# The opening of a fused attention and two-layer kernel: order of loads, places for weight tiles and keys, order of states, and idle products

## What is computed

```python
f = 1.0 / (1.0 + np.exp(-f_logit))
state = np.zeros((B, H, D, D))
for t in range(S):
    state = f[:, :, t, :, None] * state + np.einsum('bhd,bhe->bhde', k[:, :, t], v[:, :, t])
    y[:, :, t] = np.einsum('bhd,bhde->bhe', q[:, :, t], state)
x = y.transpose(0, 2, 1, 3).reshape(3072, 384)

h = x @ w_in;  g = max(h, 0) ** 2;              x2 = g @ w_out        # first layer
h = x2 @ w_in2; g = h * tanh(log1p(exp(h)));    out = g @ w_out2      # second layer
```

## Time and profile before

| | us |
|---|---|
| median of three runs | 935.17 |
| lowest and highest of them | 934.47, 936.77 |
| the profiled execution's own time | 935.64 |
| its span, first to last instruction | 933.9 |
| TensorE matmuls busy | 908.5 (97%) |
| TensorE weight loads busy | 773.7 (83%) |
| VectorE busy | 581.7 (62%) |
| ScalarE busy | 598.6 (64%) |
| GpSimd busy | 54.0 (6%) |

### The profile page before, as it was taken

How to read it: one execution, slowest core, us unless ns; L and a number is a source line. 1 busy time by engine, 2 the same in 40 slices (tenths; PEclk the granted TensorE clock), 3 DMA queues, 4 the chain that set the end, 5 groups by cost and what they waited for, 6 DMA issues and landing times.

```text
span 933.9 us, 15574 instructions
## 1 busy us (share of the span) xinstructions
PE 908.5 (97%) x5952; PEld 773.7 (83%) x5952; DVE 581.7 (62%) x1011; ACT 598.6 (64%) x1029; POOL 54.0 (6%) x48
## 2 busy tenths in 40 slices
PE   5799999999999999999999999999999999999998
PEld 3587888888878788887788799999999899999987
DVE  7656524523443443242133599898898898898886
ACT  5566654545545455553456787787787787877875
POOL 0111111101210111110000000000000000000000
PEclk9999999999999999999999999999999999999999
DMA  6533422112121121200223400200101001000000
GB/s 183 157 122 119 129 71 82 43 41 76 42 77 40 42 82 42 71 18 1 70 68 101 135 1 1 68 1 17 52 1 34 35 0 35 35 1 1 35 1 35
DMA packets 30353, 50.62 MB, mean 54 GB/s; under 512 B 3266, under 2 KB 14530, under 8 KB 30274
## 3 DMA queue, kind: packets, MB, share of 16 engines
q1 hardware_dynamic: 30274, 49.56, 17.0%
HBM read 40.11 MB, written 9.44 MB: 53 GB/s over the span
## 4 chain that ended last, share of the span: by engine, by line
PE 94%; DVE 2%; ACT 1%; issue 1%; DVEq 0%; ACTq 0%
PE ps L897 42%; PE ps L949 21%; PE ps L912 21%; PE ps L881 3%; PE ps L858 3%; PE ps L877 2%; PE ps L887 1%; PE ps L847 1%; DVE w_lo L673 0%; DVE work L711 0%; DVE work L718 0%; DVE g_lo L722 0%; DVE work L708 0%; DVE work L652 0%; ACT yo L480 0%
## 5 line engine op out<-in xcount | busy, mean ns | idle before, releaser
L897 PE MATMUL ps<-xs,w_hi 128*128 128x512 f32 x1152 | 363.7, 397 | 8.8 <-DVE w_lo L673 4.6
L897 PEld LDWEIGHTS ps<-xs,w_hi 128*128 128x128 f32 x1152 | 212.1, 188 | 53.0 <-issue 5.1
L690 DVE TENSOR_TENSOR g_lo<-gb,g_hi 128x512 fp32r<-128x512 f32 x96 | 70.2, 732 | 261.5 <-ACT gb L471 261.5
L897 PE MATMUL ps<-xs,w_lo 128*128 128x512 f32 x576 | 227.0, 394 | 0.0
L466 ACT ACTIVATE rb<-ps 128x512 f32<-128x512 f32 x96 | 57.4, 598 | 152.5 <-PE ps L897 152.5
L949 PE MATMUL ps<-w_hi,g_hi 128*128 128x384 f32 x384 | 129.4, 337 | 0.9 <-DVE g_lo L722 0.9
L949 PE MATMUL ps<-w_hi,g_lo 128*128 128x384 f32 x384 | 129.5, 337 | 0.0
L949 PE MATMUL ps<-w_lo,g_hi 128*128 128x384 f32 x384 | 128.9, 336 | 0.0
L897 PEld LDWEIGHTS ps<-xs,w_lo 128*128 128x128 f32 x576 | 108.5, 188 | 23.7
L912 PE MATMUL ps<-g_hi,w_hi 128*128 128x512 f32 x288 | 112.4, 390 | 0.0
L912 PE MATMUL ps<-g_lo,w_hi 128*128 128x512 f32 x288 | 112.3, 390 | 0.0
(11 more groups left out here) (59 smaller groups left out, 1091.0 us busy)
## 6 DMA issues: line engine op xcount, KB each, us to landing
work<-fkq SPq DMA_DIRECT2D x72, 224.0 KB, 3.7
work<-v_tok SPq DMA_DIRECT2D x24, 256.0 KB, 3.5
stage<-w_in SPq DMA_DIRECT2D x32, 192.0 KB, 2.4
stage<-w_out SPq DMA_DIRECT2D x32, 192.0 KB, 2.6
x_scratch<-yo SPq DMA_DIRECT2D x6, 768.0 KB, 3.5
xs<-x_scratch SPq DMA_DIRECT2D x6, 768.0 KB, 4.4
out<-work SPq DMA_DIRECT2D x24, 192.0 KB, 1.9
mx_scratch<-mx SPq DMA_DIRECT2D x1, 0.4 KB, 5.8
```

Source lines behind the costliest of these rows:

```text
L690: nc.vector.tensor_tensor(g_lo[:, t % 4, :], gb[:, t % 2, :], g_hi[:, t % 4, :].bitcast(F32), ALU.subtract).then_inc(s_["g1_ready"], 1)
L897: ins = nc.tensor.matmul(bank, w[:, f, k * P:(k + 1) * P], xs[:, half, part, k, :], start=k == 0 and i == 0, stop=k == KT - 1 and i == 2)
```

## The change

- SP's list has a new order, with weight tiles 0 to 3 in it. One transfer brings a whole weight tile, since the two weight matrices are laid side by side in memory.
- There are four places for the first layer's tiles: two in `stage` and two in `yo` (`w_stage`). A load of the first layer waits for the split of four tiles earlier. `w_tile(k)` is 3 + k, and a tile's load stands in the iteration before its split instead of two before.
- The transposed keys of jobs 2 and 3 go into `gb` (`key_rows`), so that `keys_out` of the first four jobs waits for no increment.
- The increments are a function of their own, called later, in banks 0, 1, 2 and 5 for jobs 0 to 3. `values` of jobs 2 and 3 wait for states 0 and 1.
- The lists of VectorE and ScalarE have a new order: the states come behind the queries, three tiles are split in the opening.
- Fourteen products of the 128x128 identity with itself stand ahead of the first keys on TensorE.

```diff
+    AHEAD = 4
+    WARM = 14
+        def kv_bank(j):
+            return (0, 1, 2, 5)[j] if j < B else 2
+
         def ps_kv(j):
-            return ps[:, a_bank(j), 0:NP * DV].rearrange("p (n c) -> p n c", c=DV)
+            return ps[:, kv_bank(j), 0:NP * DV].rearrange("p (n c) -> p n c", c=DV)
...
-            if 0 <= k < NF - 2:
-                return 2 + k
+            if 0 <= k < NF - 3:
+                return 3 + k
...
+        def w_stage(u):
+            if u < NF and u % AHEAD >= 2:
+                return u % AHEAD, yo[:, :, :].rearrange("p k t -> p (k t)")[:, WF * (u % 2):WF * (u % 2) + WF]
+            return u % 2, stage[:, u % 2, :]
+
+        def key_rows(j):
+            if j in (2, 3):
+                return gb[:, j % 2, 0:NP * R].rearrange("p (n r) -> p n r", r=R)
+            return ktT[:, j % 2, :, :]
...
             def load_w(u):
-                w_in, w_out = (w1_in, w1_out) if u < NF else (w2_in, w2_out)
-                wait(sp, s_["w_split"], u - 1)
-                sp.dma_start(stage[:, u % 2, 0:DM], w_in[u % NF]).then_inc(w_loaded[u % 2], 16)
-                sp.dma_start(stage[:, u % 2, DM:WF], w_out[u % NF]).then_inc(w_loaded[u % 2], 16)
+                w = w1 if u < NF else w2
+                wait(sp, s_["w_split"], u - AHEAD + 1 if u < NF else u - 1)
+                slot, buf = w_stage(u)
+                sp.dma_start(buf, w[u % NF]).then_inc(w_loaded[slot], 16)
...
-                if (u := w_tile(k)) is not None and u + 2 < 2 * NF and u + 2 != NF and u + 2 != NF + 1:
-                    load_w(u + 2)
+                if 0 <= k < NF - AHEAD:
+                    load_w(k + AHEAD)
...
# SP, opening
             load_f(0)
             load_f(1)
             load_k(0)
+            load_k(1)
             load_q(0)
-            load_k(1)
+            load_f(2)
             load_q(1)
+            load_f(3)
+            load_k(2)
             load_v(0)
+            load_k(3)
             load_q(2)
+            load_w(0)
             load_v(1)
-            load_f(2)
-            load_k(2)
-            load_f(3)
-            load_k(3)
             load_q(3)
-            load_w(0)
+            load_w(1)
+            load_w(2)
+            load_f(4)
+            load_k(4)
+            load_w(3)
             load_v(2)
-            load_w(1)
-            load_f(4)
             load_v(3)
-            load_k(4)
             load_q(4)
             load_v(4)
-            load_w(2)
             load_q(5)
-            load_w(3)
...
# ScalarE
             def keys_out(j):
                 act.wait_ge(s_["kT_done"], j + 1)
-                wait(act, s_["kv_done"], min(j - 1, NJ - B))
-                nc.scalar.activation(ktT[:, j % 2, :, :], ps_k(j), ACT.Copy).then_inc(s_["kT_out"], 1)
+                if j >= B:
+                    act.wait_ge(s_["kv_done"], min(j - 1, NJ - B))
+                nc.scalar.activation(key_rows(j), ps_k(j), ACT.Copy).then_inc(s_["kT_out"], 1)
...
             decay(1)
+            inverse_decay(2)
             keys_out(1)
-            inverse_decay(2)
             inverse_decay(3)
             decay(2)
             keys_out(2)
             decay(3)
-            x1_hi(0)
             keys_out(3)
             weights_hi(0)
+            x1_hi(0)
+            weights_hi(1)
             x1_hi(1)
+            weights_hi(2)
             inverse_decay(4)
             x1_hi(2)
             x1_hi(3)
-            weights_hi(1)
...
# VectorE
             first_keys(3)
-            state(0)
             first_residual(2)
...
             queries_refined(3)
+            state(0)
+            x1_lo(0)
+            mask(2)
             state(1)
-            mask(2)
-            x1_lo(0)
             x1_lo(1)
+            mask(3)
             weights_lo(0)
-            mask(3)
             x1_lo(2)
             x1_lo(3)
+            weights_lo(1)
             state(2)
             state(3)
-            weights_lo(1)
+            weights_lo(2)
...
# TensorE, values(j)
+                if j in (2, 3):
+                    pe.wait_ge(s_["s_ready"], j - 1)
...
+            def increments(j):
+                if j >= NJ - B:
+                    return
+                if j < 2:
+                    pe.wait_ge(s_["kT_out"], j + 3)
+                for n in range(NP):
+                    for par, (lo, hi) in enumerate(PAR):
+                        ins = nc.tensor.matmul(ps_kv(j)[lo:hi, n, :], key_rows(j)[:, n, lo:hi], vb[:, j % 2, 2 * n + par, :],
+                                               start=True, stop=True, skip_group_check=True)
+                ins.then_inc(s_["kv_done"], 1)
...
+            pe.wait_ge(s_["const_ready"], 2)
+            for i in range(WARM):
+                nc.tensor.matmul(ps[:, 0, 0:P], ident[:, :], ident[:, :], start=True, stop=True)
 
             keys(0)
             keys(1)
...
             keys(2)
             values(0)
             keys(3)
+            increments(0)
             scores(2)
             values(1)
+            increments(1)
             scores(3)
             values(2)
+            increments(2)
             values(3)
+            increments(3)
```

More of the change, by code:

```diff
@@ L14, with attention_ffn @@
 GAP = 64
-def attention_ffn(nc, fkq, v_tok, vT, w1_in, w1_out, w2_in, w2_out, out):
+def attention_ffn(nc, fkq, v_tok, vT, w1, w2, out):
     B, H, D, S = vT.shape
@@ L26, in attention_ffn @@
     NJ = NS * B
-    NF = w1_in.shape[0]
+    NF = w1.shape[0]
     KT = DM // P
@@ L186, in attention_ffn @@
         v_in = [sem(f"v_in{i}") for i in range(2)]
-        w_loaded = [sem(f"w_loaded{i}") for i in range(2)]
+        w_loaded = [sem(f"w_loaded{i}") for i in range(AHEAD)]
         x2_in = [sem(f"x2_in{i}") for i in range(2)]
@@ L315, in iteration @@
                     load_w(NF + 1)
+                if 0 <= k - SPLIT - 3 < NF - 2:
+                    load_w(NF + k - SPLIT - 1)
                 if k == SPLIT - 5:
@@ L453, in weights_hi @@
             def weights_hi(u):
-                act.wait_ge(w_loaded[u % 2], 32 * (u // 2 + 1))
+                slot, buf = w_stage(u)
+                act.wait_ge(w_loaded[slot], 16 * (u // AHEAD + 1 if u < NF else NF // AHEAD + (u - NF) // 2 + 1))
                 if u >= NF:
                     act.wait_ge(s_["g1_used"], SPLIT + u - NF + 1)
-                nc.scalar.activation(w_hi[:, u % NF, :], stage[:, u % 2, :], ACT.Copy).then_inc(s_["w_hi_ready"], 1)
+                nc.scalar.activation(w_hi[:, u % NF, :], buf, ACT.Copy).then_inc(s_["w_hi_ready"], 1)
             def x2_hi(c, d):
@@ L672, in weights_lo @@
                 dve.wait_ge(s_["w_hi_ready"], u + 1)
-                nc.vector.tensor_tensor(w_lo[:, u % NF, :], stage[:, u % 2, :], w_hi[:, u % NF, :].bitcast(F32),
+                nc.vector.tensor_tensor(w_lo[:, u % NF, :], w_stage(u)[1], w_hi[:, u % NF, :].bitcast(F32),
                                         ALU.subtract).then_inc(s_["w_split"], 1)
@@ L970, in iteration @@
                     values(j)
+                    increments(j)
+            pe.wait_ge(s_["const_ready"], 2)
+            for i in range(WARM):
+                nc.tensor.matmul(ps[:, 0, 0:P], ident[:, :], ident[:, :], start=True, stop=True)
             keys(0)
@@ L1018, in lay, with tiles @@
         return np.ascontiguousarray(a)
-    def tiles_in(w):
-        dm, dff = w.shape
-        return lay(w.reshape(dm // P, P, dff // P, P).transpose(2, 1, 0, 3)).reshape(dff // P, P, dm)
-    def tiles_out(w):
-        return lay(w.reshape(w.shape[0] // P, P, w.shape[1]))
+    def tiles(w_in, w_out):
+        dm, dff = w_in.shape
+        first = w_in.reshape(dm // P, P, dff // P, P).transpose(2, 1, 0, 3).reshape(dff // P, P, dm)
+        return lay(np.concatenate([first, w_out.reshape(dff // P, P, dm)], axis=2))
     b, h, s, d = q.shape
@@ L1052 @@
         "v_tok": padded(v), "vT": lay(v.transpose(0, 1, 3, 2)),
-        "w1_in": tiles_in(moe_w_in[rows]), "w1_out": tiles_out(moe_w_out),
-        "w2_in": tiles_in(moe2_w_in), "w2_out": tiles_out(moe2_w_out),
+        "w1": tiles(moe_w_in[rows], moe_w_out), "w2": tiles(moe2_w_in, moe2_w_out),
     }
```

## The result

The changed kernel takes 929.67 us (median of five runs, 928.99 to 930.41), the kernel before 934.47 in the same series (933.95 to 936.77): ratio 0.9944, 95% interval 0.9929 to 0.9958. The gain is 4.8 us where 9.5 were forecast. The direction was right; the time lies 0.4 us above the top of the range. The profiled execution took 929.81 us, its span is 928.1 (before 935.64 and 933.9).

A forecast was written before the change was run, and what follows sets the result against it. TensorE was taken as the bound after 52 us, with VectorE's order deciding what it gets before. Earlier attention 4.2, clock 2.3 and weight wait 3.5 us gave 10.0; blended with 9.2, gain 9.5: 935.17 to 925.7 us, range 924.0 to 929.3.

The forecast's parts named there:

- The sum of the opening: Before the fourth tile: VectorE's new list, shorter weight wait and higher clock start that tile at 42.1 us, 10.0 us earlier.
- The step that failed: TensorE after 52 us: its four waits, longest 1.4 us, move with its work, so earlier gains reach the end whole.
- The fifth rival: After 52 us: a wait tied to clock time gives the gain back, no change over 0.3%; chance 0.03.
- The second rival: Loop's 1.2 us hole before the third tile: TensorE's clock falls again, costing about 2.3 us, 927.9 us; chance 0.06.
- the case of 0.40: Opening: TensorE's clock is lost and returns in scores or values of jobs 1 to 3, gain 9.2 us; chance 0.40.
- third rival: Opening loads: transfers are the bound, taking 0.8 to 2 us off the gain, 926.5 to 927.7 us; chance 0.04.
- the forecast's own rows: VectorE's third scan in the opening: follows the second job's block at 13.37 us, where it started at 13.73 us before.
- Fourth rival: First layer's loop: weight tiles loaded one iteration ahead come late and make the kernel slower; chance 0.02.

The follow-up runs named there:

- e1: The changed kernel with 200 never-executed instructions added in the jumped-over body of TensorE's branch: 924.94 us, ratio 0.9889 to the kernel before.
- e4: The changed kernel with 56 never-executed instructions added in the jumped-over body of TensorE's branch: 925.23 us, ratio 0.9895.
- e3: The changed kernel without its fourteen idle products (WARM = 0): 925.11 us, ratio 0.9892.
- e2: The kernel before with 56 never-executed instructions added in the jumped-over body of TensorE's branch: 941.79 us, ratio 1.0061.
- e9: The changed kernel with 240 never-executed instructions added in the jumped-over body of TensorE's branch: 926.49 us, ratio 0.9904.
- e10: The changed kernel with 8 never-executed instructions added in the jumped-over body of TensorE's branch: 930.43 us, ratio 0.9951.
- e5: e1 with two places for weight tiles instead of four and the third split back in the loop: 930.07 us, ratio 0.9950.
- e7: e1 with the first fourteen loads in their old order and tile 0 behind them: 925.22 us, ratio 0.9895.
- e8: e3 with scan 4 on VectorE moved ahead of states 2 and 3 and the third weight split: 923.51 us, ratio 0.9877.
- e6: e1 with state 0 back ahead of the queries of job 2 on VectorE: 927.13 us, ratio 0.9915.

## Why the prediction was half right

**The sum of the opening held.** VectorE's list, the start of the layer, the hole before the third tile and its new releaser, and the fourth tile all came within 0.15 us. e1, which has no second wait at the branch, gains 10.2 us (935.13 less 924.94) where the opening's sum gave 10.0.

**The step that failed** is the sentence of the first part that each of the four waits after 52 us "hangs on work that moves with TensorE", the branch among them. The profiler put no engine behind the row of 1.4 us in the earlier trace rows, and I took it for a fixed price. It hangs on where the code behind the branch lies. The change puts 58 more instructions ahead of it (28 more matmul records and 28 more weight loads; the remaining two are semaphore records), and these moved the landing from 67 to 9 instructions before the end of a block (9 is the count of records in the trace, 67 is 9 + 58). In the profiled executions of the changed kernel and e1, whose spans are 4.7 us apart, it comes out so: the fifth product behind the landing comes 3.63 us after the first instead of 1.01, which is 2.6 us of standing; 13 products up to 457.9 us at 0.43 instead of 0.23 us each are another 2.6 us of clock; the first wait is 0.5 us shorter (0.98 against 1.47). e1, e4 and e3 take the loss away, e2 puts it into the kernel before, and e9 and e10 shift it by the count.

**The fifth rival** was the right place with the wrong cause: it asked for a wait "tied to clock time", and had a chance of 0.03. The second rival had the clock's fall, at 35 us instead of 451.

**The clock in the opening** went as in the case of 0.40: high at 7.3, low from 10.7, high again from 21 in the changed kernel's profile. But I had it return at 26 to 28, for 0.8 us lost; it returned at 21 behind keys, values and increments that stood close together from 15.66 on, and nothing was lost. When it returns is not fixed: at 19.1 to 21.1 us in the profiles of e1, e3, e4, e5, e9 and e10, at 25.5 in e7, 25.9 in e8 and 30.0 in e6. e8 shows what a late return costs, since up to there its lists are those of e3: scores 2 take 2.08 us instead of 1.16, the load of v of job 3 waits for values 1 and comes late (TensorE's wait of 0.26 us in the row under e8), and the first product of the layer starts at 31.21 instead of 30.85. e3 and e8 have no idle products, e1 and e7 have them (e7 with the old order of loads), and in each pair one return is early and one late. So they neither held the clock nor brought it back. Whether the transposes were the reason that it fell isn't decided (the forecast cites the Trainium skill, "TensorE: Matmul & The Clock Gate", section "Part 4: PE-mode transpose", by which they don't count as busy): two groups of them were all that ran between the idle products and 11.45 in the changed kernel, where it fell at 10.7, but in e1's profile, with the same code, the first scores still ran at the high clock and only the second were slow:

```profile
11.43 1.16 PE L883 MATMUL ps<-work 48*128 48x128 f32 x16 [1.41 <-DVE work L675]
13.51 2.08 PE L883 MATMUL ps<-work 48*128 48x128 f32 x16 [0.91 <-DVE work L675]
```

**Loads.** Transfers were not the bound in the changed kernel (third rival), but the slack of v of job 3 is thin: in e7 and e8, where the clock came back late, TensorE waits 0.21 and 0.26 us for it. e7 gives the order of the loads 0.3 us, near the 0.4 us that the forecast's own rows gave (13.73 against 13.37); it isn't clear of the noise. The name of the change puts the loads first; on the path they are the least of it.

**What the parts are worth**, on e1: four places 5.1 us (hole and clock), state 0 behind the queries 2.2, load order 0.3, idle products 0.2. The sum is 7.8 of 10.2, and the parts need not add up; the first three compare two series, and by the ratios they are 5.7, 2.4 and 0.6. The new banks for keys and increments, and the other states and splits, were not taken out alone; what they bring stays open.

**Fourth rival.** Nothing of the late loads in the loop was seen: the waits of TensorE after 52 us are the four rows and no more.

## What to carry to other kernels

Read the start of the bound engine's dense part from the order lists and row durations; here that sum was right to 0.15 us. But a change of the instruction count ahead of a jump moves the landing behind it, so compare the waits called "issue" at each branch, and the granted clock behind them, before a gain or a loss is put down to the change. Padding that is jumped over tells the two apart, since nothing of it is executed; but its count matters, and e2 and e10 show that it can bring the loss as well as take it away. Idle products can be worth only what the stretch behind them is bound by TensorE's clock; here it was bound by VectorE, and they did not hold the clock either.

## What the runs showed of the hardware

- TensorE's code came in packets of 16 KB, one for every 255 to 257 instructions on average (the changed kernel, e1 and the kernel before, 470 to 930 us).
- Behind the taken jump TensorE went on after 0.97 (e5) to 1.47 us (e1) and ran to the end of a block; the next instruction ran 3.6 us (changed kernel), 3.8 us (e2) and 4.3 us (e9) after the restart, each time 1.3 to 1.4 us behind the end of the packet. With 65 instructions (e1, e3), 67 (the kernel before) or 209 (e4) to the end no second wait was seen.
- The packet started 0.6 us after the restart in the changed kernel and e2, and 2.0 us after it in e1 and e9; why is open. It took 1.65 and 1.87 us in the first two, 0.93 us in the others. The store of 768 KB (448.64) and the load of 768 KB behind it (450.47) leave at the same time; whether they make the packet later was not tried.
- The clock fell behind waits of 2.46 (changed kernel), 2.40 (e2), 4.58 (e5) and 4.61 us (e10, and before the third tile in the kernel before), and not behind 1.53 (e9) and 1.24 us (the third tile in the changed kernel).
- The clock column reads 1.00 until the first change of level that was recorded. In the kernel before, this hid 32 us at 1.2 GHz.
